# Attention in steps of two head pairs, its outputs in the PSUM banks of the scores, values and keys loaded apart

## What is computed

```python
# q, k, v: (8, 8, 576, 64)
scores = q @ k.T / sqrt(64)
ret = scores * Dmat                  # gamma[h] ** (i - j) where i >= j, else 0
attn = ret @ v
x = attn.transpose(0, 2, 1, 3).reshape(4608, 512)
h = maximum(maximum(x @ w1, x @ w2), x @ w3)      # w: 512 x 768
x = h @ w_out                                     # 768 x 512
h = (x @ u1) * (x @ u2) @ u3                      # 512 x 1024, u3 1024 x 1024
out = h @ u_out                                   # 1024 x 512
```

## Time and profile before

| | |
|---|---|
| runs of the kernel | 1254.2 us median of 3, 1253.05 to 1257.62 |
| profiled execution, time | 1254.5 us |
| its span | 1252.7 us |
| attention, to the first product | 182.56 us |
| TensorE busy | 98% of the span |

### The profile page before, as it was taken

How to read it: one execution, slowest core, us unless ns; L and a number is a source line. 1 busy time by engine, 2 the same in 40 slices (tenths; PEclk the granted TensorE clock), 3 DMA queues, 4 the chain that set the end, 5 groups by cost and what they waited for, 6 DMA issues and landing times. The chain is left out here.

```text
span 1252.7 us, 21052 instructions
## 1 busy us (share of the span) xinstructions
PE 1228.5 (98%) x8288; PEld 1207.5 (96%) x8288; DVE 793.2 (63%) x1194; ACT 460.0 (37%) x707; POOL 447.6 (36%) x248
## 2 busy tenths in 40 slices
PE   7999999999999999999999999999999999999999
PEld 6999989999999999998999999999999999999998
DVE  6778758755646363669599767553545365876563
ACT  2232224423323232425554535242424243555441
POOL 4576429220202020063678562202020216366540
PEclk9999999999999999999999999999999999999999
DMA  9999954020202021143555441313132243444441
GB/s 369 365 393 316 318 170 166 33 95 26 101 26 100 27 90 38 34 169 120 177 188 190 154 145 52 114 57 102 51 103 70 93 153 129 152 151 153 157 158 64
DMA packets 83075, 174.40 MB, mean 139 GB/s; under 512 B 8992, under 2 KB 57632, under 8 KB 82976
## 3 DMA queue, kind: packets, MB, share of 16 engines
q1 hardware_dynamic: 82976, 173.05, 39.2%
HBM read 109.58 MB, written 63.44 MB: 138 GB/s over the span
## 5 line engine op out<-in xcount | busy, mean ns | idle before, releaser
L972 PE MATMUL ps<-chi,whi 128*128 128x384 f32 x2016 | 676.5, 336 | 12.7 <-DVE h L809 4.6
L974 PE MATMUL ps<-chi,wlo 128*128 128x384 f32 x2016 | 674.8, 335 | 0.0
L973 PE MATMUL ps<-clo,whi 128*128 128x384 f32 x2016 | 674.6, 335 | 0.0
L522 POOL TENSOR_TENSOR raw<-raw,raw 128x768 f32<-128x768 f32 (+2 forms) x96 | 267.3, 2803 | 583.3 <-DMA raw<-x2d 207.7
L972 PEld LDWEIGHTS ps<-chi,whi 128*128 128x128 f32 x2016 | 379.5, 188 | 17.7 <-issue 8.9
L973 PEld LDWEIGHTS ps<-clo,whi 128*128 128x128 f32 x2016 | 379.7, 188 | 0.0
L974 PEld LDWEIGHTS ps<-chi,wlo 128*128 128x128 f32 x2016 | 379.4, 188 | 0.0
L721 DVE TENSOR_TENSOR clo<-raw,chi 128x768 fp32r<-128x768 f32 (+2 forms) x168 | 247.2, 1499 | 23.7 <-ACT chi L647 23.5
L647 ACT CAST chi<-raw 128x768 fp32r<-128x768 f32 (+2 forms) x168 | 180.3, 1081 | 86.8 <-PE ps L974 58.5
L714 ACT COPY w<-ps 128x384 f32<-128x384 f32 x126 | 60.6, 481 | 228.8 <-PE ps L974 227.4
L697 ACT COPY u<-ps 128x384 f32<-128x384 f32 x126 | 60.6, 481 | 171.2 <-PE ps L974 169.7
(11 more groups left out here) (41 smaller groups left out, 868.6 us busy)
## 6 DMA issues: line engine op xcount, KB each, us to landing
qks<-qk SPq DMA_DIRECT2D x32, 576.0 KB, 6.6
vks<-vk SPq DMA_DIRECT2D x32, 576.0 KB, 6.0
gd<-h SPq DMA_DIRECT2D x96, 192.0 KB, 1.9
...
raw<-hd SPq DMA_DIRECT2D x24, 576.0 KB, 5.6
...
```

The source lines that it names most:

```text
L522: return nc.gpsimd.tensor_tensor(out_, a, b, op)
L972: nc.tensor.matmul(to, w1, x1, start=(start and k == 0), stop=False, skip_group_check=True)
L973: nc.tensor.matmul(to, w1, x2, start=False, stop=False, skip_group_check=True)
L974: last = nc.tensor.matmul(to, w2, x1, start=False, stop=(k == KH[st] - 1), skip_group_check=True)
```

## The change

A step now has two head pairs: step m (0 to 16) makes scores and states of pairs 2m and 2m+1 and reads out pairs 2m-2 and 2m-1; it has two quarters. Outputs of attention are written to the banks that held the scores of the same step (0 to 3), once VectorE has read these. `vks` becomes `vs` (320 KB a pair, five buffers) and `ks` (256 KB, two). `probs` has four buffers, `vdec` and `state` two. `make_state` of both pairs waits for both sums, and the waits ahead of the products are spread over the first of them. The tables of the splits are written anew.

```diff
-STEPS = NP + 1
+STEPS = NP // 2 + 1
...
-U3_LOAD = {max(4 * kb - 2, 0): kb for kb in range(1, FT2)}
-U3_HI = {max(4 * kb, 1): kb for kb in range(FT2)}
-U3_LO = {max(4 * kb + 1, 1): kb for kb in range(FT2)}
-UO_AT = {1: 0, 2: 1, 3: 2, 4: 3}
-WC_READ = {4 * kb + 3 + WC_FROM: kb for kb in range(FT2 - 1)}
-P1_W_LOAD = {8: 0, 10: 1}
-P1_W_SUM = {10: 0, 12: 1}
-P1_W_HI = {11: 0, 14: 1}
-P1_W_LO = {12: (0, 0), 14: (0, 1), 15: (1, 0), 16: (1, 1)}
-P1_RAW = 12
-P1_T = {15: 0, 16: 1, 17: 2, 18: 3}
-P1_HI = {18: 0, 19: 1, 20: 2, 22: 3}
-P1_LO = {19: 0, 20: 1, 22: 2, 23: 3}
...
+def made_in(m):
+    return [n for n in (2 * m, 2 * m + 1) if n < NP]
+
+
+def read_in(m):
+    return [n for n in (2 * m - 2, 2 * m - 1) if n >= 0]
+
...
+def quarters(m):
+    if m == STEPS - 1:
+        return range(2 * (m - WC_FROM), QUARTERS)
+    return range(2 * (m - WC_FROM), 2 * (m - WC_FROM) + 2) if m >= WC_FROM else ()
...
+U3_LOAD = {2 * kb: kb for kb in range(FT2)}
+U3_SPLIT = {2 * kb + 1: kb for kb in range(FT2)}
+UO_LOAD = {0: (0, 1), 1: (2, 3)}
+UO_SPLIT = {1: (0, 1), 2: (2, 3)}
+WC_READ = {2 * kb + 1 + WC_FROM: kb for kb in range(FT2 - 1)}
+WC_READ[STEPS - 1] = FT2 - 1
+P1_W_LOAD = {4: 0, 5: 1}
+P1_W_SUM = {5: 0, 6: 1}
+P1_W_HI = {6: 0, 7: 1}
+P1_W_LO = {6: ((0, 0),), 7: ((0, 1), (1, 0)), 8: ((1, 1),)}
+P1_RAW = 6
+P1_T = {7: (0, 1), 8: (2, 3)}
+P1_HI = {9: (0, 1), 10: (2, 3)}
+P1_LO = {9: (0,), 10: (1, 2), 11: (3,)}
...
+        vs = [at(f"vs{i}", [P, V_COLS], f32, v_at + i * V_COLS * 4) for i in range(5)]
+        ks = [at(f"ks{i}", [P, K_COLS], f32, k_at + i * K_COLS * 4) for i in range(2)]
+        p_at = H_AT + 4 * N * 4
+        probs = [at(f"probs{i}", [P, 2, SEQ], f32, (o, o + 2 * SEQ * 4, p_at, p_at + 2 * SEQ * 4)[i])
+                 for i in range(4)]
...
+        S_TAIL = (4, 5)
+        S_STATE, S_WC = 6, 7
...
+            def load_v(n):
+                if n >= 5:
+                    sp.wait_ge(valued, n - 4)
+                sp.dma_start(vs[n % 5][:, :], vv[n, :, :]).then_inc(v_loaded[n % 5], 16)
+
+            def load_k(n):
+                if n >= 2:
+                    sp.wait_ge(state_summed, n - 1)
+                sp.dma_start(ks[n % 2][:, :], kk[n, :, :]).then_inc(k_loaded[n % 2], 16)
...
             load_qk(0)
-            sp.dma_start(vtab[:, :, :], vdecay).then_inc(vtab_loaded, 16)
-            load_vk(0)
-            sp.dma_start(dec[:, 0:2, :], decay[:, 0:2, :]).then_inc(dec_loaded[0], 16)
+            sp.dma_start(vtab[:, 0:2, :], vdecay[:, 0:2, :]).then_inc(vtab_loaded[0], 16)
+            load_v(0)
+            sp.dma_start(dec[:, 0:4, :], decay[:, 0:4, :]).then_inc(dec_loaded[0], 16)
             load_qk(1)
+            load_k(0)
+            load_v(1)
+            load_k(1)
+            load_qk(2)
             sp.dma_start(qtab[:, :, :], qdecay).then_inc(qtab_loaded, 16)
-            load_vk(1)
-            sp.dma_start(dec[:, 2:HEADS, :], decay[:, 2:HEADS, :]).then_inc(dec_loaded[1], 16)
-            load_u3(0)
-            load_uo(0)
-            load_qk(2)
-            load_vk(2)
-            load_uo(1)
-            for n in range(STEPS):
-                if n + 3 < NP:
-                    load_qk(n + 3)
-                if n in U3_LOAD:
-                    load_u3(U3_LOAD[n])
-                if n in (1, 2):
-                    load_uo(n + 1)
-                if n in P1_W_LOAD:
-                    load_weight(P1_W_LOAD[n])
-                if n == P1_RAW:
+            load_v(2)
+            load_qk(3)
+            sp.dma_start(dec[:, 4:HEADS, :], decay[:, 4:HEADS, :]).then_inc(dec_loaded[1], 16)
+            sp.dma_start(vtab[:, 2:PAIRS, :], vdecay[:, 2:PAIRS, :]).then_inc(vtab_loaded[1], 16)
+            load_v(3)
+            load_v(4)
+            for m in range(STEPS):
+                if m in U3_LOAD and m < STEPS - 2:
+                    load_u3(U3_LOAD[m])
+                for i in UO_LOAD.get(m, ()):
+                    load_uo(i)
+                if m in P1_W_LOAD:
+                    load_weight(P1_W_LOAD[m])
+                if m == P1_RAW:
                     load_raw(0)
-                if n + 3 < NP:
-                    load_vk(n + 3)
-                if n >= 1:
-                    store_x(n - 1)
-                if n - 1 in WC_READ:
-                    store_wc(WC_READ[n - 1])
-            store_wc(FT2 - 1)
+                if 2 * m + 4 < NP:
+                    load_qk(2 * m + 4)
+                for n in (2 * m + 2, 2 * m + 3):
+                    if n < NP:
+                        load_k(n)
+                if m >= 1 and 2 * m + 3 < NP:
+                    load_v(2 * m + 3)
+                if 2 * m + 5 < NP:
+                    load_qk(2 * m + 5)
+                if m >= 1:
+                    store_x(2 * m - 2)
+                    if 2 * m + 4 < NP:
+                        load_v(2 * m + 4)
+                    store_x(2 * m - 1)
+                if m in WC_READ:
+                    store_wc(WC_READ[m])
 
...
-                    pool.wait_ge(vtab_loaded, 16)
-                else:
-                    pool.wait_ge(state_summed, n)
-                add(vdec[:, :, :], vks[n % 4][:, 0:NC * CH].rearrange("p (n c) -> p n c", c=P),
+                pool.wait_ge(v_loaded[n % 5], 16 * (n // 5 + 1))
+                if n in (0, 2):
+                    pool.wait_ge(vtab_loaded[n // 2], 16)
+                if n >= 2:
+                    pool.wait_ge(state_summed, n - 1)
...
-            decay_values(0)
-            for n in range(NP):
-                decay_queries(n)
-                if n + 1 < NP:
-                    decay_values(n + 1)
-                if n in P1_W_SUM:
-                    sum_weight(P1_W_SUM[n])
-                if n in P1_T:
-                    combine(0, P1_T[n])
+            for n in made_in(0):
+                decay_values(n)
+            for m in range(STEPS - 1):
+                for n in made_in(m):
+                    decay_queries(n)
+                for n in made_in(m + 1):
+                    decay_values(n)
+                if m in P1_W_SUM:
+                    sum_weight(P1_W_SUM[m])
+                for i in P1_T.get(m, ()):
+                    combine(0, i)
...
+            for m in range(STEPS):
+                if m in U3_SPLIT:
+                    split_u3(U3_SPLIT[m])
+                for i in UO_SPLIT.get(m, ()):
+                    split_uo(i)
+                if m in WC_READ:
+                    read_wc(WC_READ[m])
+                for n in read_in(m):
+                    read_values(n)
+                if m in P1_W_HI:
+                    split_weight(P1_W_HI[m], 0)
+                    split_weight(P1_W_HI[m], 1)
+                for pos in P1_HI.get(m, ()):
+                    split_tokens(0, pos)
...
-                if n >= 2:
-                    dve.wait_ge(valued, n - 1)
+                if n in (0, 2):
+                    dve.wait_ge(dec_loaded[n // 2], 16)
+                if n >= 4:
+                    dve.wait_ge(valued, n - 3)
                 for h in range(2):
                     nc.vector.tensor_tensor(
-                        probs[:, n % 2, h, 0:NC * CH].rearrange("p (n c) -> p n c", c=CH),
-                        ps[:, h, :].rearrange("p (n c) -> p n c", c=CH),
+                        probs[n % 4][:, h, 0:NC * CH].rearrange("p (n c) -> p n c", c=CH),
+                        ps[:, 2 * (n % 2) + h, :].rearrange("p (n c) -> p n c", c=CH),
                         dec[:, 2 * p + h, :].unsqueeze(1).broadcast_to([P, NC, CH]), ALU.mult).then_inc(decayed, 1)
+
+            def decay_tail(n):
+                p = n % PAIRS
+                dve.wait_ge(scored, n + 2 - n % 2)
                 nc.vector.tensor_tensor(
-                    probs[TAIL:P, n % 2, :, NC * CH:SEQ], ps[TAIL:P, S_TAIL[0]:S_TAIL[1] + 1, 0:TAIL],
+                    probs[n % 4][TAIL:P, :, NC * CH:SEQ],
+                    ps[TAIL:P, S_TAIL[0]:S_TAIL[1] + 1, (n % 2) * TAIL:(n % 2 + 1) * TAIL],
                     dec[TAIL:P, 2 * p:2 * p + 2, TAIL:CH], ALU.mult).then_inc(decayed, 1)
...
-                dve.wait_ge(state_summed, n + 1)
+                dve.wait_ge(state_summed, n + 2 - n % 2)
...
+            for m in range(STEPS):
+                for n in made_in(m):
                     decay_scores(n)
-                if n in U3_LO:
-                    split_u3(U3_LO[n])
-                if n in UO_AT:
-                    split_uo(UO_AT[n])
-                if n in P1_W_LO:
-                    split_weight(*P1_W_LO[n])
-                if n in P1_LO:
-                    split_tokens(0, P1_LO[n])
-                if n < NP:
+                for n in made_in(m):
+                    decay_tail(n)
+                if m in U3_SPLIT:
+                    split_u3(U3_SPLIT[m])
+                for i in UO_SPLIT.get(m, ()):
+                    split_uo(i)
+                for wi, part in P1_W_LO.get(m, ()):
+                    split_weight(wi, part)
+                for pos in P1_LO.get(m, ()):
```

(49 more changed lines are left out.)

124 lines of the change are left out of this document (51 added, 73 removed).

## The result

The change makes the kernel slower: 1283.17 us (median of 6 runs, 1280.61 to 1287.08) against 1253.62 us, ratio 1.0232 with a 95% interval of 1.0208 to 1.0257. The direction was predicted, the size was not: 1266 us was forecast, with a range up to 1274, and the time lies 9 us above that range. The profiled execution took 1280.6 us, its span is 1278.8 us; the one before took 1254.5 us. The 26.1 us between them are what has to be explained.

The account below looks back on a forecast made before the run. TensorE was taken to bound attention, with no waits in its steps. From 1254.5 us: shapes -8.7, start +4.3, hand-over -1.2, low parts +13.0, clock +5 gave 1266.9, stated as 1266; own range 1261 to 1271, whole range 1252 to 1274.

Parts of the forecast that it names:

- term 6: Attention: extra waits of scores on output reads, VectorE's work, single cast buffers and GpSimd's work, all costed at nothing.
- term 4: Steps 7, 8, 10, 11: query_state waits for VectorE, held by low parts behind late casts; 3.2 us each, +13.0.
- term 5: TensorE's clock falls to half behind the four stalls and the wait in step 1; 1.0 us each, +5.
- the start: Step 1: sum_state(2) waits some 3 us for keys landing at 24.2, step 2 starts at 27.5; +4.3 us.
- term 1: Attention steps 2 to 15: half the changes of tile shape, 0.62 us saved per double step of 9.98; -8.7 us.
- the hand-over: From attention to the products: TensorE's 1.39 us wait for the last quarter row goes, a shape change stays; -1.2 us.
- the second rival: Late loads of values, chained through GpSimd's list, make a 13 us loop against 9.98; 1270 us, chance 0.12.
- such waits as a sign of being wrong: Attention: the prediction is wrong if TensorE waits in the steady steps for vdec, the decayed values; no size given.
- The rival with the low parts free: VectorE reaches the next step's table in time, low parts cost nothing; 1249.9 us, or 1246.5; chance 0.18.
- half the stalls: Only half of the low-part stalls occur, say the weights' two are covered; 1258 us, chance 0.10.
- the clock that stays up: The stalls occur but TensorE's clock does not fall, adding 0 or 1 us; 1261.9 to 1263 us, chance 0.14.

Follow-up runs that it names:

- e7: e5 with the changed kernel's own tables of low parts (cast and low part in one double step); 1274.5 us, ratio to before 1.0145.
- e8: Kernel before with the hand-over alone: last quarter row read ahead of last outputs, waits moved to the products overwriting those banks; 1254.8 us, ratio 0.9995.
- e1: Changed kernel with low parts of weights and token blocks one double step behind their casts; 1278.5 us, ratio to before 1.0185.
- e5: e1 with GpSimd's weight sums and token combinations moved ahead of the decayed values, plus a sixth buffer of values; 1260.6 us, ratio to before 1.0040.
- e9: e5 with one wait more in the products: GpSimd's first combination for the last token tile waits for VectorE's low parts; 1256.8 us, ratio to before 1.0005.

## Why the prediction was wrong

Its sum was 1254.5 - 8.7 + 4.3 - 1.2 + 13.0 + 5 = 1266.9. By the measured terms it is 1254.5 - 6.6 + 6.2 - 1.4 + 24.4 + 3.6 = 1280.7, and the profiled execution took 1280.6. The 24.4 us are what is left over in the steps, so that this sum closes is no proof; the experiments are.

**The step that failed** is in term 6: the loop of the late loads of values was put at nothing, as hidden behind term 4. It added 7.6 us on top of term 4 (24.4 with it, 16.8 without it in e7). Terms 4 and 5 without the start stand for 17.0 us of the sum, so 7.4 of the 13.8 us between 1266.9 and 1280.7 come from there, 3.6 from the products, 2.1 from term 1 and 0.9 from the start, less 0.2 at the hand-over.

1. *Changes of shape*, -8.7: right in kind, too large. A double step takes 10.12 us, not 9.98, so 0.47 and not 0.62 are saved, 14 x 0.47 = 6.6. The quiet step above against twice (10.14 for 10.60) shows where the rest went: scores save 0.15 (2.37 for 2.52) where 0.26 were counted, quarters 0.12 for 0.11, queries and sums together 0.10 (1.82 for 1.86, 0.98 for 1.04) for 0.16, values 0.09 as counted. So two groups of scores side by side keep a part of the holes between them.
2. *Start*, +4.3: the place and the wait were right (24.79 for 24.2 us, 3.58 for some 3 us), the size was not. Step 2 starts at 29.42 and not 27.5, so +6.2. From 24.79 to 29.40 us the granted clock was 0.63, which is some 1.7 us of the 1.9; 1 us for it stood in term 5.
3. *Hand-over*, -1.2: right. No bracket at 205.06, and e8 shows 1.45 from pair 30 on.
4. *Low parts*, +13.0: right, place by place. By themselves they cost 12.7 us (e7). In the changed kernel the four waits are 2.57 to 3.39 us where 2.8 was predicted: the four low parts took 1.38, 1.74, 1.59 and 0.96 us and not 1.05. The terms as listed add up to T + 8.1, not 8.0.
5. *Clock*, +5: right in size. It is 4.9 us behind the first three of the four stalls, none behind the fourth, and some 1.7 in step 1; in e7 it is 4.1 us for the four stalls. The rule of the Trainium skill named there ("TensorE: Matmul & The Clock Gate", section "A second HAM failure mode: psum-queue depth-cycling"), read as each wait paid in full, is not borne out here: in e7 the clock stayed up behind two of the four waits, and one of these was the longest.
6. *Costed at nothing*: this is where it failed, and with it the second rival. The loop through GpSimd and the loads of values was seen, its turn worked out as 13 us (13.7 measured in e1), and its loss put at 10 us, "hidden by the 2.4 us of margin and the 13 us of term 4". By itself the chain costs 16.2 us (the 19.2 of e1 less the 3.0 that e5 keeps); term 4 with its clock costs 16.8 by itself (e7, which loses nothing outside its four steps). Both together cost 24.4, so 7.6 of the chain show. Against e7, step by step, the changed kernel loses 4.6 us in steps in which e7 loses nothing, 3.9 more in steps 7 and 8, and 0.9 less in steps 10 and 11. The clock makes little of the 7.6: it costs 4.9 against 4.1 us. So the chain is late in other steps than term 4 too (`sum_state` waits at 68.51 and 121.70 us in the changed kernel, and the prediction had named such waits as a sign of being wrong). Within one step, by the order of the waits, a stall in `query_state` moves the values' end, and so the issue of the next values, as far as it moves their use; this was argued, not measured by itself. Two waits in one loop hide each other only in part; I treated the longer as cover for the shorter. The cover of 0.5 us for scores on the read of outputs was thin too: scores wait 0.62 us for it once here and 1.8 us in e5.

A seventh term was missing: +3.6 in the products, net, with an order between GpSimd and VectorE 900 us behind the edit as its main part.

The rival with the low parts free is out (e7), and so are half the stalls and the clock that stays up. The idea of the change saves no time here even with all this mended: e9 has two-pair steps with 2.5 us of loss left and ties with before (1.0005). The 6.6 us of shapes and 1.4 us of hand-over go to the start and to that loss, and no version here beat the kernel before by more than the measurement tells.
